# Routed experts on one core: half of each hidden tile turned by DMA in 16-bit planes

## The reference

```python
N, D, E, F = (4608, 512, 8, 1024)
for e in range(E):
    mask = expert_idx == e
    h = np.maximum(x[mask] @ w1[e], 0.0)
    out[mask] = gate_w[mask, None] * (h @ w2[e])
```

## Time and profile before

| | us |
|---|---|
| median of 3 runs | 1445.52 |
| lowest, highest | 1443.98, 1447.59 |
| the profiled execution, device time | 1442.98 |
| its span (the records' first start to last end) | 1441.2 |
| TensorE busy | 1427.0 (99%) |
| VectorE, ScalarE, GpSimd busy | 779.8, 569.0, 663.4 |

### The profile page before, as it was taken

One profiled execution on the slowest core, in us unless ns is written; L12 is line 12 of the kernel. 1 busy time (PEld: TensorE's weight loads), 2 busy tenths in 40 slices (PEclk: granted clock), 3 DMA queues, 4 the chain that ended last, 5 costly groups with the idle time before them and its releaser, 6 DMA issues.

```text
span 1441.2 us, 21909 instructions
## 1 busy us (share of the span) xinstructions
PE 1427.0 (99%) x7617; PEld 1180.7 (82%) x7617; DVE 779.8 (54%) x1498; ACT 569.0 (39%) x1012; POOL 663.4 (46%) x619
## 2 busy tenths in 40 slices
PE   8999999999999999999999999999999999999998
PEld 7888888888888888888888888888888888888886
DVE  6656777676667767676666575770002800055550
ACT  5333332222232232322222322545555555555553
POOL 5552244253252352442232232475555755577763
PEclk9999999999999999999999999999999999999999
DMA  8534131131131231211110122262222742237330
GB/s 247 168 117 153 39 102 58 34 105 45 46 95 49 58 107 30 76 63 30 59 45 15 38 95 74 89 225 69 71 69 55 232 135 68 55 114 232 117 97 13
DMA packets 106409, 129.24 MB, mean 90 GB/s; under 512 B 48828, under 2 KB 65212, under 8 KB 106176
## 3 DMA queue, kind: packets, MB, share of 16 engines
q1 hardware_dynamic: 59200, 99.20, 22.0%
q0 software_dynamic: 8032, 18.93, 4.2%
q10 hardware_dynamic: 39072, 9.70, 3.6%
HBM read 92.34 MB, written 29.43 MB: 84 GB/s over the span
## 4 chain that ended last, share of the span: by engine, by line
PE 94%; DVE 2%; ACT 1%; issue 1%; DMA 1%; POOL 1%; SPq 0%; ACTq 0%; POOLq 0%; DVEq 0%
PE y_ps L817 26%; PE h_ps L801 25%; PE y_ps L956 16%; PE y_ps L923 16%; PE h_ps L935 3%; PE h_ps L761 3%; PE step_ps L720 2%; PE step_ps L740 2%; DMA emb_all<-in_v 1%; DVE rank_in_list L1182 0%; ACT L1409 0%; DVE shared L1032 0%; POOL g_lo L1720 0%; DMA y_rows<-in_k 0%; DVE g_full L1109 0%
## 5 line engine op out<-in xcount | busy, mean ns | idle before, releaser
L1720 POOL TENSOR_TENSOR g_lo<-g_full,g_hi 128x512 fp32r<-128x512 f32 x144 | 192.7, 1339 | 516.3 <-ACT g_hi L1452 516.3
L801 PE MATMUL h_ps<-x_hi_in,weight_parts 128*128 128x512 f32 x1144 | 376.3, 392 | 0.0
L817 PE MATMUL y_ps<-weight_parts,g_hi 128*128 128x512 f32 x1152 | 359.7, 393 | 0.3 <-POOL g_lo L1720 0.3
L1452 ACT ACTIVATE g_hi<-g_full 128x512 fp32r<-128x512 f32 x144 | 91.1, 632 | 517.0 <-PE y_ps L817 413.7
L801 PEld LDWEIGHTS h_ps<-x_hi_in,weight_parts 128*128 128x128 f32 x1144 | 214.8, 188 | 43.9
L817 PEld LDWEIGHTS y_ps<-weight_parts,g_hi 128*128 128x128 f32 x1152 | 213.1, 188 | 45.6 <-POOL g_lo L1720 0.7
L923 PE MATMUL y_ps<-weight_parts,x_hi_in 128*128 (+1 forms) x1032 | 242.0, 390 | 0.0
L923 PEld LDWEIGHTS y_ps<-weight_parts,x_hi_in 128*128 128x128 f32 x1032 | 193.3, 188 | 40.5 <-issue 0.6
L817 PE MATMUL y_ps<-weight_parts,g_lo 128*128 128x512 f32 x576 | 224.6, 390 | 0.0
L801 PE MATMUL h_ps<-x_lo_in,weight_parts 128*128 128x512 f32 x572 | 222.8, 390 | 0.0
L1109 DVE TENSOR_SCALAR g_full<-h_ps,alpha 128x512 f32<-128x512 f32 x144 | 107.7, 748 | 193.8 <-PE h_ps L801 192.2
(11 more groups left out here) (212 smaller groups left out, 1738.6 us busy)
## 6 DMA issues: line engine op xcount, KB each, us to landing
shared<-in_w SPq DMA_DIRECT2D x8, 2048.0 KB, 9.3
emb_all<-in_w SPq DMA_DIRECT2D x8, 2048.0 KB, 9.5
y_dram<-y_rows SPq DMA_DIRECT2D x9, 1024.0 KB, 4.3
shared<-in_q SPq DMA_DIRECT2D x34, 256.0 KB, 3.0
shared<-in_v SPq DMA_DIRECT2D x29, 288.0 KB
x_dram<-shared SPq DMA_DIRECT2D x32, 256.0 KB, 3.3
y_rows<-x_dram SPq DMA_DIRECT2D x32, 256.0 KB, 3.2
shared<-in_k SPq DMA_DIRECT2D x26, 288.0 KB, 2.9
```

Of the source, the lines that this page charges most:

```text
L801: mm = pe.matmul(h_ps[:, f % 2, :], w[:, k, f * P:(f + 1) * P], x[:, k, :], start=(n == 0), stop=(n == 3 * DC - 1))
L817: mm = pe.matmul(y_ps[:, j, :], a[:, f % 2, j * P:(j + 1) * P], w[:, f, :], start=(f == 0 and n == 0), stop=(f == FC - 1 and n == 2))
L1452: act.activation(gh[:, f % 2, :], g_full[:, f % 2, :], ACT.Copy).then_inc(gh_done, 1)
L1720: pool.tensor_tensor(gl[:, f % 2, :], g_full[:, f % 2, :], gh[:, f % 2, :].bitcast(F32), ALU.subtract).then_inc(gl_done, 1)
```

## The change

From slot 6 on the first half (h = 0) of the hidden tile takes the way that the input rows already take. `turn_hidden` (ScalarE) stands where `hidden(n, 0)` was: it parts the half in PSUM, before the ReLU, in two 16-bit planes in SBUF and issues a DMA transpose of both. `join_hidden` (ScalarE) stands behind `hidden_columns(n, 1)`: it joins the turned words and makes the hi part with a ReLU. On GpSimd `hidden_lo(n, 0)` becomes two instructions, the ReLU of the joined tile and the subtraction. The two SBUF tiles used are `hs` columns 0 to 511 and the first half of `ht`, by turns. `turn_h(n, 0)` and `hidden_columns(n, 0)` fall away. Layer two of such a slot sums the chunks of h = 1 first and those of h = 0 after them. To make room on ScalarE, `part_rows` moves to GpSimd, at the head of its round; the DMA issue behind it stays on ScalarE (`turn_rows`).

```diff
+            if n >= BY_DMA and h == 0:
+                return h0_lo_done, n - BY_DMA + 1
...
             def slot_layer2(n, found, turns=True):
...
-                for f in range(EFC):
+                for step in range(EFC):
+                    f = step if n < BY_DMA else (step + HALF) % EFC
...
-                    if turns and f == 1:
+                    if turns and step == 1:
...
-                        turn_h(n + 1, 0)
+                        if n + 1 < BY_DMA:
+                            turn_h(n + 1, 0)
                         turn_h(n + 1, 1)
...
-            def part_rows(n):
-
+            def turn_rows(n):
 
                 m = n - BY_DMA
...
+                act.wait_ge(parted, 2 * (m + 1))
+                if m:
                     act.wait_ge(joined, 2 * m)
...
+            def turn_hidden(n):
+
+
+                m = n - BY_DMA
+                here, there = h0_bufs[m % 2], h0_bufs[(m + 1) % 2]
+                act.wait_ge(hr_done, 2 * n + 1)
...
+                for w in range(2):
+                    act.activation(planes[:, w, :], bits[:, :, w], ACT.Copy).then_inc(h0_parted, 1)
+                act.wait_ge(h0_parted, 2 * (m + 1))
+                if m:
+                    act.wait_ge(h0_hi_done, m)
+                act.wait_ge(*ht_lo_ready(n - 1, 0))
+                act.dma_start(out=there.bitcast(U16).rearrange("p (k n) -> p k n", n=P),
+                              in_=here.bitcast(U16), transpose=True).then_inc(h0_planes_turned, 16)
+
+            def join_hidden(n):
...
+                act.wait_ge(h0_planes_turned, 16 * (m + 1))
...
+                for w in range(2):
+                    act.activation(bits[:, :, w], planes[:, w, :], ACT.Copy).then_inc(h0_joined, 1)
+                act.wait_ge(h0_joined, 2 * (m + 1))
+                act.activation(ht_part(n, 0, 0), here.rearrange("p (b n) -> p b n", n=P),
+                               ACT.Relu).then_inc(h0_hi_done, 1)
...
+            def part_rows(n):
+
+                m = n - BY_DMA
+                pool.wait_ge(gathered[n % AHEAD], 16 * (n // AHEAD + 1))
...
+                for w in range(2):
+                    pool.tensor_copy(halves[:, w, :], bits[:, :, w]).then_inc(parted, 1)
...
+                    pool.wait_ge(h0_hi_done, n - BY_DMA + 1)
+                    pool.tensor_scalar(here, here, 0.0, None, ALU.max).then_inc(h0_relu_done, 1)
+                    pool.wait_ge(h0_relu_done, n - BY_DMA + 1)
+                    pool.tensor_tensor(ht_part(n, 0, 1), here, ht_part(n, 0, 0).bitcast(F32),
+                                       ALU.subtract).then_inc(h0_lo_done, 1)
+                    return
...
             for n in range(EARLY, NSLOT):
+                if BY_DMA <= n + 2 < NSLOT:
+                    part_rows(n + 2)
                 if n + 1 < NSLOT:
                     columns_lo(n + 1)
-                hidden_lo(n, 0)
-                hidden_lo(n, 1)
+                hidden_lo(n, 0 if n < BY_DMA else 1)
+                hidden_lo(n, 1 if n < BY_DMA else 0)
                 scatter(n - 1)
```

More of the change, by code:

```diff
@@ L297, in stages, with by_pe, hidden_read @@
         ht = y[:, 2:4, :].rearrange("p a (b n) -> p (a b) n", n=P)
+        h0_bufs = (hs[:, 0:512], ht[:, 0:HALF, :].rearrange("p b n -> p (b n)"))
         def ht_part(n, h, part):
             return ht_parts[n % 2][part][:, h * HALF:(h + 1) * HALF, :]
+        def by_pe(n, h):
+            return 2 * n + h + 1 if n < BY_DMA else BY_DMA + n + 1
         def ht_lo_ready(n, h):
-            return (ht_lo_done, 2 * (n - 1) + h + 1) if n else (first_ht_lo, h + 1)
+            if n >= BY_DMA and h == 0:
+                return h0_lo_done, n - BY_DMA + 1
+            return (ht_lo_done, by_pe(n, h) - 2) if n else (first_ht_lo, h + 1)
+        def hidden_read(n, h):
+            if n >= BY_DMA and h == 0:
+                return h0_parted, 2 * (n - BY_DMA + 1)
+            return hr_copied, by_pe(n, h)
         stage2 = emb[:, :, :].rearrange("p e n -> p (e n)")
@@ L1533, in part_rows @@
                     act.wait_ge(joined, 2 * m)
[L1534 to L1537, removed]
                 act.dma_start(out=halves_t.rearrange("p w (k n) -> p (w k) n", n=P),
                               in_=halves.rearrange("p w n -> p (w n)"), transpose=True).then_inc(halves_turned, 16)
+            def turn_hidden(n):
+                m = n - BY_DMA
+                here, there = h0_bufs[m % 2], h0_bufs[(m + 1) % 2]
+                act.wait_ge(hr_done, 2 * n + 1)
+                if m == 0:
+                    act.wait_ge(h_turned, by_pe(n - 1, 0))
+                else:
+                    act.wait_ge(h0_joined, 2 * m)
+                bits = hr_ps[:, 0, :].bitcast(U16).rearrange("p (n w) -> p n w", w=2)
+                planes = here.bitcast(U16).rearrange("p (w n) -> p w n", w=2)
+                for w in range(2):
[6 more added lines that the diff above has]
+                              in_=here.bitcast(U16), transpose=True).then_inc(h0_planes_turned, 16)
@@ new lines, in join_hidden @@
+            def join_hidden(n):
+                m = n - BY_DMA
+                here, there = h0_bufs[m % 2], h0_bufs[(m + 1) % 2]
+                act.wait_ge(h0_planes_turned, 16 * (m + 1))
+                bits = here.bitcast(U16).rearrange("p (n w) -> p n w", w=2)
+                planes = there.bitcast(U16).rearrange("p (w n) -> p w n", w=2)
+                for w in range(2):
[3 more added lines that the diff above has]
+                               ACT.Relu).then_inc(h0_hi_done, 1)
@@ L1647, in _ @@
             for n in range(1, NSLOT):
-                hidden(n, 0)
+                if n < BY_DMA:
+                    hidden(n, 0)
+                else:
+                    turn_hidden(n)
                 hidden(n, 1)
@@ L1654, in _ @@
                 if BY_DMA <= n + 2 < NSLOT:
-                    part_rows(n + 2)
-                hidden_columns(n, 0)
+                    turn_rows(n + 2)
+                if n < BY_DMA:
+                    hidden_columns(n, 0)
                 if n + 1 == EARLY:
@@ L1659, in _ @@
                 hidden_columns(n, 1)
+                if n >= BY_DMA:
+                    join_hidden(n)
                 finish(n - 1)
@@ L1781, in hidden_lo @@
             def hidden_lo(n, h):
-                pool.wait_ge(ht_hi_done, 2 * n + h + 1)
+                if n >= BY_DMA and h == 0:
+                    here = h0_bufs[n % 2].rearrange("p (b n) -> p b n", n=P)
+                    pool.wait_ge(h0_hi_done, n - BY_DMA + 1)
[4 more added lines that the diff above has]
+                    return
+                pool.wait_ge(ht_hi_done, by_pe(n, h))
                 pool.tensor_tensor(ht_part(n, h, 1), ht[:, h * HALF:(h + 1) * HALF, :], ht_part(n, h, 0).bitcast(F32),
```

28 lines of the change are left out of this document (16 added, 12 removed).

## The result

The changed kernel takes **1492.08 us** (median of 3 runs, 1491.68 to 1493.74) against 1445.52 before: 46.6 us or 3.2% slower, ratio 1.0324 with a 95% interval of 1.030 to 1.0348. That is on the side that was forecast and inside the range, but nearly twice the forecast loss of 25.5 us.

A forecast was written before the change was run, and what follows sets the result against it. TensorE, busy 99% of the span, was taken to bound the kernel. Transposes removed -16.1, ring hindered by VectorE's splitting +36.6, late landings +5: +25.5 us on 1442.98, giving 1468.5, or 1471 us as median; range 1432 to 1510.

The forecast's parts named there:

- What bounds it, and the gain: TensorE bounds slots 6 to 42; four fewer transposes in each save 0.435 us, 16.1 us in all, leaving 11.345 us slots.
- the price of GpSimd's ReLU: GpSimd's ReLU over 512 columns, like its two 16-bit copies, was taken at 0.61 us, between bounds of 0.29 and 1.28.
- The free ring: GpSimd and ScalarE work in series between last subtractions of successive slots, VectorE idle: 11.02 us against TensorE's 11.345, no loss.
- The rival with slow instructions: New GpSimd instructions at 0.9 us each exceed TensorE's slot everywhere, giving 1490 us; at 1.28 each, 1528; chance 0.15.
- The hindered ring: The GpSimd and ScalarE series while VectorE splits weights: 16.92 us, 5.58 over TensorE's slot, losing 36.6 us in all.
- a short stretch: VectorE's first weight splitting of an expert, 10.8 us long, three in the changed slots: 1.8 us lost in each.
- the long one: VectorE's next weight splitting of an expert, 31.5 us long, three in the changed slots: 10.4 us lost in each.
- The rival that only GpSimd's work counts in the stretches: While VectorE splits weights, rounds overlap and GpSimd's own work sets 14.26 us a round: 1456 us, chance 0.10.
- Its own signs: Expected free slots of 11.35 us, 14 to 17 during splitting; wrong if long-stretch slots stay under 12 or free exceed 11.5.
- A reading: From the profile before: VectorE's copy, hindered by GpSimd's subtraction of 1107.06, needs 1.78 us and ends with it.
- Landings: DMA transposes outside the stretches that meet a 2 MB weight load land late; two or so cost TensorE 5 us.
- ScalarE has room: ScalarE gets 1.9 us more work a slot against 3.56 us idle less 0.435, so it alone has room.

## Why the prediction was right in direction and short in size

The measured terms, from differences of medians: the transposes -17.1 (neither splitting nor loads, ReLU on ScalarE, against before); GpSimd's ReLU +23.7; the loads +6.2 (1457.66 - 1451.46), or 7.7 when taken from the other end; VectorE +34.4 (1492.08 - 1457.66). They sum to +47.2, which is no test: each term ends where the next begins, and the sum is 1492.08 less the 1444.92 of the kernel before in the last group. Nor do they simply add: moving the ReLU gains 23.7 us undisturbed and 30.4 in the whole kernel. Beside them the prediction had -16.1, 0, +5 and +36.6.

- **What bounds it, and the gain.** Right: 16.1 forecast, 17.1 measured once nothing disturbs, slots at 11.37 (11.345 forecast).
- **The step that was mis-sized: the price of GpSimd's ReLU.** "512 columns are estimated at 0.61 us" was taken for all three new instructions. It holds for the copies (0.602 at least, 0.59 each when in a pair) and not for the ReLU, a TENSOR_SCALAR: 1.49 us. That is above even the upper bound I gave, 1.28, the two-input subtraction. The slope came from a cast and an affine select, other operations, and an operation's price doesn't follow from another's with as many inputs.
- **The free ring.** 11.02 us plus the missing 0.88 is 11.90; measured 11.96. The prediction had "0.32 us to spare", and so made the term for free slots zero. It was the thinnest margin of the sum. The rival with slow instructions put a ring of 11.89 at 1490 us: its number was nearly the measured one, though by three instructions of 0.9 instead of two of 0.59 and one of 1.49.
- **The hindered ring.** 16.92 forecast; 16.2 in the changed kernel, 16.4 and 15.9 without loads. The loss for it, 36.6, was 34.4, and that near agreement is partly luck. Without loads a short stretch costs one slot of 15.2 us, 3.2 above the free slots where 1.8 had been counted, and the long one shown two of 16.4 and 15.9, 8.3 above where 10.4 had been; the slowed ring was taken too long and the slots in the short stretches too short. Part of the 34.4 is the clock and not the ring (last section), and part of the waiting is ahead of layer one, a place that the prediction did not price. The 1.00 us charged for a hindered copy was close (2.70 for two, against 2 x 1.41). The rival that only GpSimd's work counts in the stretches is out: 14.26 us were not seen in the changed kernel, and order alone moved 26 us.
- **Its own signs.** "I am wrong if [...] the free slots are above 11.5": they are at 11.97, so by that sign the account failed for the free slots, and for the reason above. In the long stretch GpSimd was busy 26.83 of 31.5 us (1133.0 to 1164.5), 85% and not the 90% or more of the list. The rest of the list held: slots of 15.2 to 18.3 us while VectorE splits, TensorE's waits ahead of the transposes ended by the ReLU copy of half 1, copies of 0.59 us when free and 1.35 when not.
- **A reading.** VectorE's copy begun at 1108.16 does not end with GpSimd's subtraction, as the prediction says: the subtraction ends at 1109.39, the copy at 1109.94. No term rests on it.
- **Landings.** 5 forecast, 6 to 8 measured.
- **ScalarE has room.** Right, also with the ReLU on top. Parting from PSUM takes 1.08 for two, 1.14 was taken.
- **The Trainium skill** (SBUF — State Buffer, "Who interferes with whom"): the runs agree that it is the shared access to SBUF and not VectorE's being busy, since with VectorE as busy in PSUM GpSimd's copies stay at 614 ns. Its 769 ns for a one-input loop of 512 elements (GPSIMD Engine Reference, "Elementwise — side-by-side cycle accounting") fits neither of the two forms here, 0.59 and 1.49 us.

## What to carry to other kernels

When work moves to another engine, look for the ring it closes: add up what lies in series between two passes of the same instruction, across engines, and compare that with the bounding engine's period. A ring that is 3% shorter than the period, as this one was on paper, leaves less room than one wrong price can take (0.88 us here), and its length depends on the order in which an engine takes its work as much as on the amount. And an experiment that takes work away from one engine may let another's transfers bunch up: keep the pace when you take away the cost.

## What the runs showed that I had not expected

- On GpSimd a ReLU as TENSOR_SCALAR over 128x512 float32, in place, takes 1.49 us, more than a two-input subtraction of the same size (1.28), and 2.5 times a 16-bit copy of 512 columns (0.59).
- ScalarE's own time for issuing a DMA transpose, 1.25 us, rose to 7.31 us while two weight loads of 2 MB were in flight, and all its compute stood behind it.
- TensorE's granted clock fell in the long stretches. The changed kernel's first one (the last three columns are the granted clock, the DMA share and GB/s):

```profile
1135.00:1180.00 45.00, 33.84 (x141) 26.47 (x140) 28.83 (x23) 20.08 (x35) 34.42 (x30) 0.93 0.76 204
```

It was busy 33.84 of 45 us there, and granted 0.93 of full speed on the mean; the eighteen matmuls at 1175.47, right behind a wait of 3.56 us, took 6.85 us instead of 4.38. So a wait of TensorE here can cost more than its length.
- Not all of the 46.6 us lies in the slots that were changed. The clock was at its lower level (1.2 GHz, 0.50 of full) also from 925 to 935 us, ahead of the changed slots and with TensorE busy 9.44 of the 10 us before it. First the changed kernel, then the kernel before:

```profile
925.00:935.00 10.00, 10.00 (x41) 8.51 (x40) 4.13 (x21) 4.13 (x8) 1.27 (x1) 0.50 0.38 152
925.00:935.00 10.00, 9.54 (x61) 7.87 (x60) 7.46 (x32) 6.51 (x12) 2.47 (x2) 1.00 0.38 154
```

The first `finish` behind it starts 4.0 us later (948.26, against 944.26 before). The kernel with VectorE in PSUM had the full clock there. Why it fell there is open: the same drop is in the profiled execution of some kernels with the change (the loads cut, for one) and not of others. The other two executions of the changed kernel had the same mean clock, 0.989 and 0.988, so they may have had the drop too; no trace shows it.

An estimate of the clock's part in the 34.4 us: in slices of 15 us from 960 us on, the changed kernel's clock is below 1.00 in six (0.77, 0.96, 0.93 and three times 0.89), together 10.1 us of full clock missing; with VectorE in PSUM it is so in one ahead of the end (0.77, 3.5 us). With the 4.0 us from ahead of the slots that makes some 10 us at the most. Busy time shows the same thing more roughly: TensorE's 7469 matmuls are 1434.7 us in the changed kernel and 1411.6 in the undisturbed one with the ReLU on ScalarE. No run held the clock while it kept the waits, so how much it is stays open.
